# Expert groups among the last attention units, one weight quarter loaded later, and a new order at the change of layers

## The reference, cut to what matters

```python
# attention, 4 batches x 8 heads x 576 positions x 64
q_d, k_d, v_d = means of q, k, v over groups of 4 positions
out_d     = softmax(q_d @ k_d.T / 8) @ v_d                    # 144 x 144
out_local = softmax(mask(q @ k.T / 8, |i - j| < 4)) @ v       # a band
x  = repeat(out_d, 4) + out_local                             # 2304 x 512
# first expert layer, 512 -> 2048 -> 512
h  = x @ w_in
x  = (h * tanh(softplus(h))) @ w_out
# second expert layer, 512 -> 1024 -> 512
h  = x @ w_in2
s  = h * softmax(h)
x  = ((s - mean(s)) / sqrt(var(s) + 1e-6) * g_ln) @ w_out2
```

## Time and profile before

| | before |
|---|---|
| median of 3 runs | 716.09 us (715.68 to 717.92) |
| profiled execution, own time | 720.33 us |
| its span, first to last instruction | 718.5 us |
| busy PE / PEld / DVE / ACT / POOL | 687.0 / 635.4 / 369.5 / 263.2 / 184.9 us |
| mean granted TensorE clock | 0.983 of full speed |

### The profile page before, as it was taken

How to read it: one execution, slowest core, us unless ns; L and a number is a source line. 1 busy time by engine, 2 the same in 40 slices (tenths; PEclk the granted TensorE clock), 3 DMA queues, 4 the chain that set the end, 5 groups by cost and what they waited for, 6 DMA issues and landing times.

```text
span 718.5 us, 12623 instructions
## 1 busy us (share of the span) xinstructions
PE 687.0 (96%) x5098; PEld 635.4 (88%) x5098; DVE 369.5 (51%) x686; ACT 263.2 (37%) x583; POOL 184.9 (26%) x228
## 2 busy tenths in 40 slices
PE   6879879999999999999999999999879999999998
PEld 5767779999999999999999999999758888888886
DVE  7988957543233223322232332664886667666671
ACT  5868755332112111221121122134653445444441
POOL 5988920000000000000000000574535433454100
PEclk9988989999999999999999999999999999999999
DMA  8987983000000000000000030003000000000001
GB/s 227 246 222 207 248 300 115 0 1 1 1 1 1 0 1 1 1 1 0 1 1 1 1 117 1 1 1 89 30 1 30 29 31 15 16 30 29 31 16 44
DMA packets 24185, 37.51 MB, mean 52 GB/s; under 512 B 2624, under 2 KB 12864, under 8 KB 24000
## 3 DMA queue, kind: packets, MB, share of 16 engines
q1 hardware_dynamic: 24128, 36.71, 17.5%
HBM read 31.99 MB, written 4.72 MB: 51 GB/s over the span
## 4 chain that ended last, share of the span: by engine, by line
PE 81%; POOL 8%; DVE 4%; issue 4%; ACT 2%; DMA 1%; SPq 0%; POOLq 0%; ACTq 0%; DVEq 0%
PE psum L668 28%; PE psum L682 27%; PE psum L772 12%; PE psum L749 11%; POOL half_v L495 2%; PE psum L758 2%; POOL half_qk L482 2%; POOL prob L503 1%; POOL vd L496 1%; POOL qd L485 1%; DMA kT<-kT_dram 1%; DVE so L1272 1%; DVE wlo L1205 1%; POOL kd L485 0%; ACT ex L973 0%
## 5 line engine op out<-in xcount | busy, mean ns | idle before, releaser
L1169 DVE CAST ghi<-g_sb 128x384 fp32r<-128x384 f32 x96 | 39.7, 414 | 246.1 <-PE psum L682 189.2
L887 ACT ACTIVATE g_sb<-psum 128x384 f32<-128x384 f32 x96 | 47.2, 492 | 295.9 <-PE psum L668 292.3
L668 PE MATMUL psum<-xhi,whi 128*128 128x384 f32 x384 | 130.5, 340 | 1.7 <-issue 1.1
L668 PE MATMUL psum<-xlo,whi 128*128 128x384 f32 x384 | 130.1, 339 | 0.0
L668 PE MATMUL psum<-xhi,wlo 128*128 128x384 f32 x384 | 130.0, 338 | 0.0
L682 PE MATMUL psum<-ghi,wlo 128*128 128x384 f32 x384 | 129.0, 336 | 0.0
L682 PE MATMUL psum<-ghi,whi 128*128 128x384 f32 x384 | 129.0, 336 | 0.0
L682 PE MATMUL psum<-glo,whi 128*128 128x384 f32 x384 | 129.0, 336 | 0.0
L518 POOL TENSOR_TENSOR t<-raw 128x1024 f32<-128x1024 f32 x1 | 2.6, 2642 | 356.6 <-PE psum L682 356.6
L668 PEld LDWEIGHTS psum<-xhi,whi 128*128 128x128 f32 x384 | 73.0, 190 | 2.5 <-issue 1.7
L668 PEld LDWEIGHTS psum<-xlo,whi 128*128 128x128 f32 x384 | 73.0, 190 | 0.0
(11 more groups left out here) (121 smaller groups left out, 1067.6 us busy)
## 6 DMA issues: line engine op xcount, KB each, us to landing
wraw<-w_dram SPq DMA_DIRECT2D x12, 512.0 KB, 5.0
qT<-qT_dram SPq DMA_DIRECT2D x16, 288.0 KB, 4.6
kT<-kT_dram SPq DMA_DIRECT2D x16, 288.0 KB, 6.0
v<-v_dram SPq DMA_DIRECT2D x16, 288.0 KB
out_dram<-ob SPq DMA_DIRECT2D x18, 256.0 KB, 2.0
vw<-v_dram SPq DMA_DIRECT2D x32, 128.0 KB, 3.7
wraw<-w_dram SPq DMA_DIRECT2D x16, 256.0 KB, 5.7
raw<-w_dram SPq DMA_DIRECT2D x1, 2048.0 KB, 7.3
```

Of the source, the lines that this page charges most:

```text
L668: ins = nc.tensor.matmul(bank, a[:, w], b[:, kdx, :], start=(kdx == 0 and n == 0), stop=(kdx == KD - 1 and n == 2))
L887: nc.scalar.activation(g_sb[:, f % HR, :], psum[:, HB1 + f % HB, 0:N1], ACT.Mish).then_inc(g_ok, 1)
L1169: nc.vector.tensor_copy(ghi[:, f % GR, :], g_sb[:, f % HR, :]).then_inc(ghi_ok, 1)
```

## The change: what it does

At the first seam PE's groups of tile 0 are spread: piece 0 stands between the turning of unit 14 and the values of unit 14, piece 1 after those values, piece 2 between the turning and the values of unit 15. The fourth input chunk is added on DVE at the end of round 14 (one round earlier) and cast and subtracted in round 15. Weight piece 0, 1 and 2 are split in rounds 14, 15 and 16, one each. ACT loads the table for `mish` after the eviction of unit 14. SP no longer puts the four transfers of the second quarter of `w_in` between the last units' loads but starts them after all of these.

At the second seam ACT loads the table of the exponential first, splits four of the eight blocks of `w_out2` around `copy_p1(0)`, and turns `square(1)` behind `high2(0)`, and `out_copy(0)` and `high2(1)` ahead of `square(2)`. DVE follows with the low parts, puts the last two behind the first two row maxima, and `low2(0)` ahead of the last two combinations of pair 1.

```diff
-        ADDED = [c * BATCH + LATE + 1 for c in range(KD)]
+        ADDED = [c * BATCH + LATE + 1 for c in range(KD - 1)]
...
-                if UNITS - 2 <= s < UNITS + 2:
-                    for c in range(2 * (s - UNITS + 2), 2 * (s - UNITS + 3)):
-                        load_w_in(c // KD, c % KD)
+                if UNITS - 2 <= s < UNITS:
+                    for kdx in range(2 * (s - UNITS + 2), 2 * (s - UNITS + 3)):
+                        load_w_in(0, kdx)
+            for kdx in range(KD):
+                load_w_in(1, kdx)
             load_w_out(0)
...
+                if u == UNITS:
+                    pe.wait_ge(l_sub, UNITS)
+                if u >= UNITS:
+                    hidden(0, 2 * (u - UNITS))
                 if u >= LATE:
                     value_pooled(u - LATE)
                     value_local(u - LATE)
-
                 if u == UNITS:
-                    pe.wait_ge(l_sub, UNITS)
-                    for f in range(HB):
-                        hidden(0, f)
+                    hidden(0, 1)
...
-                if u == UNITS:
-                    nc.scalar.preload_act_table_set("mish")
-                    weights_in_high(1)
-                    evict_pooled(u - LATE)
                 if 0 < u <= UNITS:
                     normalise_pooled(u - 1)
-                if LATE <= u != UNITS:
+                if u == UNITS - 1:
+                    split_x(0, KD - 1)
+                    weights_in_high(1)
+                if u >= LATE:
                     evict_pooled(u - LATE)
...
-                if u == UNITS - 1:
+                if u == UNITS - 2:
                     weights_in_high(0)
                 if u == UNITS:
+                    nc.scalar.preload_act_table_set("mish")
                     mish(0, 0)
                     weights_in_high(2)
...
+            nc.scalar.preload_act_table_set("natural_log_exp_and_others")
+            act.wait_ge(ld_g, 16)
+            for c in range(2):
+                weights_two_out(c)
             copy_p1(0)
-            nc.scalar.preload_act_table_set("natural_log_exp_and_others")
+            for c in range(2, 4):
+                weights_two_out(c)
             tokens_high(1, 0, NPR)
...
+                    if u == UNITS - 1:
+                        split_x(0, KD - 1)
                     sum_local(u)
...
-                if u == UNITS:
-                    split_x(0, KD - 1)
-                    weights_in_low(0)
-                    weights_in_low(1)
...
+                if u == UNITS - 2:
+                    add_pooled(0, KD - 1)
+                if u >= UNITS - 2 and u <= UNITS:
+                    weights_in_low(u - UNITS + 2)
```

More of the change, by code:

```diff
@@ L702, in _ @@
                 if u == UNITS:
-                    pe.wait_ge(l_sub, UNITS)
-                    for f in range(HB):
-                        hidden(0, f)
+                    hidden(0, 1)
             for t in range(T1):
                 for f in range(F1):
-                    if t > 0 or f >= HB:
+                    if t > 0 or f >= AHEAD:
                         hidden(t, f)
@@ L997, in _ @@
                 weights_two_in(n)
+            nc.scalar.preload_act_table_set("natural_log_exp_and_others")
+            act.wait_ge(ld_g, 16)
+            for c in range(2):
+                weights_two_out(c)
             copy_p1(0)
-            nc.scalar.preload_act_table_set("natural_log_exp_and_others")
+            for c in range(2, 4):
+                weights_two_out(c)
             tokens_high(1, 0, NPR)
-            act.wait_ge(ld_g, 16)
-            for c in range(F2 - 2):
+            for c in range(4, F2 - 2):
                 weights_two_out(c)
@@ L1011, in _ @@
             square(0)
+            high2(0)
             square(1)
-            high2(0)
             tokens_high(2, 0, NPR)
@@ L1016, in _ @@
             softmax(3)
+            out_copy(0)
+            high2(1)
             square(2)
-            high2(1)
-            out_copy(0)
             copy_p1(2)
@@ L1124, in add_pooled @@
                     dve.wait_ge(od_ok, c * BATCH + 1)
+                    dve.wait_ge(x_ok, c * BATCH + 1)
                 x = xy[:, c, t * N1:(t + 1) * N1].rearrange("p (i r) -> p i r", r=POOLF)
@@ L1162, in _ @@
                     evict_local(u - LATE, 1)
-                if u == UNITS:
-                    weights_in_low(2)
+                if u == UNITS - 2:
+                    add_pooled(0, KD - 1)
+                if u >= UNITS - 2 and u <= UNITS:
+                    weights_in_low(u - UNITS + 2)
             def high(t, f):
@@ L1293, in _ @@
                 low_in(n)
+            for c in range(2):
+                low_out(c)
             add_p6(0)
-            for c in range(3):
+            for c in range(2, 4):
                 low_out(c)
@@ L1298, in _ @@
             add_p7(0)
-            for c in range(3, F2 - 2):
-                low_out(c)
+            low_out(4)
             make_c22(0)
@@ L1303, in _ @@
             make_c21(0)
-            low_out(F2 - 2)
-            low_out(F2 - 1)
+            low_out(5)
             make_c12(0)
@@ L1308, in _ @@
             softmax_max(1)
+            for c in range(F2 - 2, F2):
+                low_out(c)
             add_p6(1)
@@ L1317, in _ @@
             solu(1)
+            low2(0)
             make_c21(1)
+            make_c12(1)
             variance(1)
-            make_c12(1)
-            low2(0)
             layernorm(1)
```

## The result

The changed kernel takes 713.87 us (median of 20 runs, 709.37 to 718.65), the kernel before beside it 718.93 (20 runs, 713.90 to 721.86): ratio 0.9944, 95% interval [0.9925, 0.9964], 4.0 us faster by the ratio. The profiled execution took 714.52 us (span 712.7) where that of before took 720.33.

What follows compares the result with a forecast made beforehand. PE was taken to bound the kernel, with its waits and slow-clock stretches at the two seams; gains of 1.8 + 4.5 = 6.3 us took the median from 716.09 to 709.8, range 705.4 to 713.1, to 713.6 for rival 2.

Steps and rivals of the forecast that it cites:

- the 6.3 forecast: Whole kernel: total gain in us, 1.8 from the first seam plus 4.5 from the second.
- the 1.8: First seam: net gain of 1.8 us, piece 3 3.3 earlier less a slow stretch of 1.5; bounds 0.8 to 4.2.
- the 3.3 us: First seam: piece 3 starts at 105.95 instead of 109.23, after PE stands still for 2.66 us.
- PE's idle time hides all of this: First seam: unit 15's maxima start 0.9 us late on DVE, at no cost, since PE is busy until 91.84 either way.
- the slow stretch behind the idle 2.70: First seam, ahead of piece 3: PE idle 2.66 us, then one stretch at the lower clock costing 1.5 us.
- The 0.9 forecast ahead of piece 1: First seam: PE waits 0.9 us after unit 14's values until piece 1's low part is ready at 96.3.
- rival 1: Both seams: no slow stretch after unit 15's values, short second-seam waits; gain 4.2 + 5.5 = 9.7, so 706.4 us; chance 0.15.
- 4.5: Second seam: gain of 4.5 us, PE's waits 3.75 against 6.7 + 1.5 = 8.2 before; bounds 2.2 to 6.5.
- The forecast waits: Second seam, PE: 1.3 for `add_p6`, 0.2 product 5, 1.0 first layer norm, 0.15 `output2(0)`, 1.0 products (2,0) and (2,1).
- Rival 2: Gain of one seam only, by a new slow stretch or DVE port waits: 2.2 + 0.8 = 3.0, 713.1 us; chance 0.17.
- Rival 3: Both seams: no measurable change, because the waits are paid elsewhere; 715 to 717 us; chance 0.06.
- Rival 4: First seam: slower, because the second quarter of `w_in` lands too late for piece 4; 720 us or so; chance 0.05.

Runs made afterwards that it cites:

- the quarter early: The changed kernel with the second quarter of `w_in` loaded among the last units' loads as before the change; 712.61 us (6 runs), ratio 0.9902.
- the first seam alone: The kernel before with only the change's edits to attention rounds 14 to 17 and `w_in`, the second seam as before; 719.0 us (12 runs), ratio 0.9974.

## Why the prediction came out as it did

**The level it started from failed.** "By the same difference it goes from 716.09 to 709.8" took the median of three runs for the kernel's level, and the 4.2 us between it and the profiled execution for a fixed difference. Twenty runs of before have 718.93, 2.8 us more, and the profiled execution of the change lies 0.65 above the median of its runs. From 718.93 the same sum gives 712.6, in a range of 708.2 to 716.4. The gain, 4.0 us (2.6 to 5.4 by its interval) against the 6.3 forecast, and 6.4 with eight runs beside 19 of before, lies inside the 2.5 to 10.7 that the range gave; the time, 713.87, does not lie in the range. That the profiled execution came near its forecast (714.52, forecast 714.0) is partly luck: in it attention up to the end of unit 14's turning was 1.6 us shorter than before (90.25 against 91.84), and that moment lies anywhere between 88.5 and 93.0 in the twelve profiles. The spread of the runs goes largely with the clock. Over the runs of all kernels, one level for each kernel, a run takes 0.38 us (standard error 0.03) more for each us at the lower level, and 1.4 us of scatter is left; the slope takes up nearly six tenths of the variance. Among the changed kernel's runs, 2.8 us at the lower level go with 709.96, 21.5 us with 718.65. That is a regression over runs; it does not say which stretch was slow in which run.

**First seam: the 1.8 is not seen.** The order of the steps was right. That piece 3 started at 105.77 where 105.95 was forecast is luck, since errors in both directions met. What counts is the first output group behind it, and there nothing is left in this profile: from the end of unit 14's turning to its first matmul it is 22.4 us (90.25 to 112.67), in the profile of before 21.6 (91.84 to 113.47). Single executions differ: the change profiled again and the one with the quarter early have 20.5 and 19.4, the first seam alone 17.4, and three others with the old order 19.0 to 20.8. The means of the four each, 19.9 and 20.4, differ by less than the spread, so 1.8 is neither shown nor excluded.

What the profile does show is where the sum was wrong. Of the 3.3 us that piece 3 was to start earlier, 2.7 are the slow stretch in the profile of before: its first 24 matmuls took 6.84 (96.23 to 103.07) instead of 4.16, and the sum put all groups of the new order ahead of piece 3 at full clock. Three sizes were off.

First, the addition was put at 0.55 and took 1.34; with the piece at its upper bound the maxima came at 89.17, 3.4 us behind the start of the eviction's second half (85.74), where the forecast had 2.35 (87.05 to 89.4). "PE's idle time hides all of this" failed by that: piece 0 did not start directly behind the turning but 0.65 later, since it waits for unit 15's differences, which the sum left out. In the Trainium skill "SBUF — State Buffer", section "SBUF: two separate sides", VectorE and GpSimd lock a shared pair of ports for a whole instruction; the trace agrees for both instructions (1.34 and 1.75 beside POOL's 1.26 and 1.58), so the rule should have been applied to the addition as well.

Second, piece 0 was put at full clock and ran at half, 1.8 us more. Third, the slow stretch behind the idle 2.70 was put at 1.5; in this profile 24 matmuls took 7.07 instead of 4.40, 2.7 more, so 1.2 more than the sum had. The 0.9 forecast ahead of piece 1 did not come. Together 0.65 + 1.8 + 1.2 - 0.9 = 2.8, and the first output group came 0.8 us later instead of 1.8 earlier, a difference of 2.6.

The slow stretch isn't the same in each execution, as the chains of waits of two kernels with the same 2.70 show. The change, profiled again:

```profile
105.96 5.97 PE psum L671 x24
```

and the first seam alone:

```profile
104.17 4.40 PE psum L671 x24
```

The change with the quarter early has 5.97 too. So a slow stretch followed in three of four profiles, and in the fourth none, as rival 1 had it. The forecast argued from one execution that 2.66 is longer than the 2.27 with a slow stretch and than the 1.91 without one; in the first seam alone it is the other way round, none behind 2.70 and one behind 1.89:

```profile
525.16 0.50 PE L777 MATMUL psum<-whi,lhi 128*128 128x512 f32 x1 [1.89 <-DVE llo L1255]
526.46 0.63 PE L777 MATMUL psum<-whi,llo 128*128 128x512 f32 x1
```

What the idle time costs on average is seen in the runs: giving it a group brings 5.1 us by medians. An estimate from the rows and the slope above: 2.70 - 0.72 - 0.41 = 1.6 us of idle time, and 11.4 - 2.8 = 8.6 us less at the lower level, times 0.38 = 3.3; 4.9 together.

**Second seam: 4.5 was about right.** In the profiles, from the first product (498.72 and 497.91) to the second `turn2` (535.87 and 530.59) it is 37.15 us before and 32.68 after, 4.5 less, and to the third (547.15 and 541.16) 5.2 less; alone it is worth 6.5 us in time by medians (ratio's interval 4.4 to 9.4). The forecast waits came as 1.07 (1.3), 0 (0.2), 0.63 (1.0), 0 (0.15) and 1.15 (1.0); product 6 started nearly at once, and no slow stretch followed the 1.07. That the runs gain more than the profile's 4.5 fits the clock: 19.1 us at the lower level became 10.4.

**The rivals.** Rival 2, one seam only, describes where the gain was, though not by its reason: the second seam kept all of its gain, and for the first none can be measured on top of it. That its 713.1 lies near 713.87 is luck, since it too was counted from 716.09. Rival 3 is out by the interval. Rival 4, slower by the late second quarter, is refuted: late 0.9911, early 0.9902, each with an interval of 0.003 to either side; an effect of a microsecond or two of the quarter's place is not excluded.

Two of the prediction's figures follow from no row: the 5.5 that rival 1 gives the second seam, and the end of the range at 713.6, where rival 2's own sum is 713.1.

**What stays open.** Why the clock fell after 2.70 us in some executions and not in others, no run tells, nor why piece 0 ran at half clock behind 0.65 of idle time in one profile and at full clock behind the same 0.65 in the change profiled again:

```profile
91.94 0.45 PE L671 MATMUL psum<-xhi,whi 128*128 128x384 f32 x1 [0.65 <-DVE prob L1101]
94.40 0.72 PE L642 MATMUL psum<-pprobT,vd 72*64 72x144 f32 x8
```

What the first seam of the change is worth by itself, between nothing and some 2 us, stays open as well.

## What to carry to other kernels

A matmul group that is moved forward out of an idle gap takes its cover with it: look what runs where it stood, and price the gap that opens with the slow clock behind it, not by its length alone. Where no useful work fits, useless matmuls can keep the clock (0.997 for eight of them). A level read from three runs of a kernel that spreads over 8 us is uncertain by some 3; predict the difference and give the level its own width.

## What was not expected of the hardware

- Idle time of the same length (2.70 us) was followed by 24 matmuls in 4.40, 5.97, 5.97 and 7.07 us in four profiles.
- Time at the lower level goes with more than half of the variance between runs of one kernel: before had 7.1 to 27.4 us of it per run in 47 runs.
- A VectorE addition with two SBUF inputs went from 0.55 to 1.34 us when POOL's 1.26 us product ran beside it.
